# Expert blocks of an attention and mixture-of-experts kernel: x turned by transfers and VectorE in place of TensorE

## The chip, the cores and the metric

One Trainium2 chip, one of its cores. The metric is the time of one execution in microseconds (us), the median of several. PE is TensorE, DVE is VectorE, ACT is ScalarE, POOL is GpSimd, SP is SyncE, which here only issues DMAs.

## What is computed

Attention without softmax, then a dense layer pair, then a routed expert layer:

```python
kv = np.einsum('bhsd,bhse->bhde', k, v)                 # 8 batches, 8 heads, 576 rows, 64 wide
out = np.einsum('bhsd,bhde->bhse', q, kv)
out = out / np.sqrt(np.mean(out * out, -1, keepdims=True) + 1e-06) * g_norm
x = out.transpose(0, 2, 1, 3).reshape(4608, 512)
h = x @ w_in                                            # 512 x 2048
x = (np.maximum(h, 0) + alpha * np.minimum(h, 0)) @ w_out
logits = x @ w_gate                                     # 8 experts
e_idx = np.argmax(logits, axis=1)
for e in range(8):                                      # w1[e] 512 x 1024, w2[e] 1024 x 512
    mask = e_idx == e
    ye = np.maximum(x[mask] @ w1[e], 0) @ w2[e]
    out[mask] = gate_w[mask, None] * eom[mask, e, None] * ye
```

`gate_w` is the softmax weight of the chosen expert and `eom` a sigmoid of a second gate. All is float32. Each product is made of three: an operand is split into a high part, which the matmul's operand type holds, and the rest, and high x high, high x low and low x high are added up.

## The kernel before, in words

**Stages.** Twelve tiles of 384 tokens pass through attention and the dense pair (lines 1334 and 1346 are the latter's matmuls). Each tile writes its rows to `rows` in HBM, 512 values and 16 of metadata a token, and the token's number into the list of its expert (`lists`, line 532). Then come the *expert units*: 128 tokens of one expert each, 41 of them in this execution. Units 0 to 3 are written out one by one, between the last tile's routing and the building of a table (`tab`) of units; units from 4 on run in a hardware loop, two per round (`over_units`, L311), with slots r = 0 and 1.

**A unit.** SP loads 128 token numbers (`uid`, L424). GpSimd gathers these rows into `xrow[:, r]` (L550). PE transposes x in four 128x128 blocks into the PSUM bank psQ (`x_units`, L1429), since the matmul wants the 512 model values on partitions. ACT copies psQ to the high part of `uxT` (L731), DVE subtracts for the low part (L1144) and copies the tokens' gate and number into `umeta` (L1148). `h_unit` (L1448) makes the hidden values in two halves of 512, 12 matmuls each. ACT applies relu (L737), PE transposes h (`h_transpose`, L1458), ACT and DVE split it (`ut`: L742, L1153), and `y_unit` (L1469) adds up y in psAcc0, two halves of 12 matmuls. ACT scales y (L750) and GpSimd scatters the 128 rows to the output (L558).

**Order.** It is written out by hand, the same for all engines. PE's unit u is: h_transpose half 0, h_unit half 1, x_units of unit u+1, y_unit half 0, h_transpose half 1, h_unit half 0 of unit u+1, y_unit half 1. DVE's is ut half 0, ux of u+1 (L1144, L1148), a part of the weights' split (`expert_low`, L966), ut half 1, the other parts. GpSimd's is: wait until x of unit u is transposed and its metadata read, gather for unit u+2, scatter of unit u. Engines meet by semaphores; each engine's instructions start in the order written, so what stands behind a waiting instruction waits too.

**Weights.** An expert's w1 and w2 come in four pieces each of 128x1024 (L406, L409: 512 KB, on SP's queue) into four buffers (`stage2`), and ACT and DVE split them into `W` (L725, L966). w1's piece ch holds the 128 model rows from 128 ch on.

## Time and profile before

| | us |
|---|---|
| three runs, median | 1503.25 |
| lowest and highest | 1499.38, 1505.24 |
| the profiled execution | 1500.92 |
| its span, first to last instruction | 1499.1 |
| PE busy | 1468.6 |
| DVE, ACT, POOL busy | 723.5, 491.3, 127.6 |
| granted clock of TensorE, mean | 0.994 |

The profile is of one execution. Its page gives busy times, a chain of work followed back from the last instruction, and groups of instructions by line; the trace behind it can be asked for a timeline, for one line's instructions and for stretches. Start times count from the first instruction. The rows that count here stand in a section below.

### The profile page before, as it was taken

To read this page: it belongs to the slowest core of one execution; us is meant where nothing else is said; L and a number is where in the kernel's file an instruction comes from. 1 tells how busy PE (TensorE), PEld (TensorE's weight loads), DVE (VectorE), ACT (ScalarE), POOL (GpSimd) and SP (SyncE) were. 2 spreads that over 40 slices of the span, in tenths; PEclk is the share of its full clock that TensorE was granted. 3 is DMA by queue.
4 is the path that set the end of the run, shared out by engine and by line. 5 is a ranking of instruction groups with operands and counts; after the bars stand their busy time and mean duration, and the time that the engine had idled before them with its cause. 6 is when DMAs were issued, how large, how long until landed. Compare 5 with 4: busy or idle time off the path is not lost.

```text
span 1499.1 us, 27268 instructions
## 1 busy us (share of the span) xinstructions
PE 1468.6 (98%) x8553; PEld 1277.5 (85%) x8554; DVE 723.5 (48%) x1796; ACT 491.3 (33%) x994; POOL 127.6 (9%) x143
## 2 busy tenths in 40 slices
PE   7899999999999999999999999999999999999997
PEld 6788989888898989898989898887888888888886
DVE  3585555565656465645555655663122114444411
ACT  3442232323232323223222221433233234444422
POOL 1000000000000000000000000112111111111111
PEclk8999999999999999999999999999999999999999
DMA  8532121102121102213100000524123114444410
GB/s 193 136 95 70 33 75 33 43 2 75 33 75 33 43 2 61 46 36 71 31 13 23 1 22 1 146 88 156 44 91 106 43 37 149 155 142 157 152 41 32
DMA packets 100516, 104.51 MB, mean 70 GB/s; under 512 B 55296, under 2 KB 75920, under 8 KB 100434
## 3 DMA queue, kind: packets, MB, share of 16 engines
q1 hardware_dynamic: 91618, 80.99, 19.6%
q0 software_dynamic: 7872, 21.09, 4.4%
q10 hardware_dynamic: 944, 1.33, 0.4%
q8 instruction: 53, 0.87, 0.3%
q14 instruction: 29, 0.24, 0.1%
HBM read 84.04 MB, written 20.65 MB: 70 GB/s over the span
## 4 chain that ended last, share of the span: by engine, by line
PE 90%; DMA 4%; DVE 2%; ACT 1%; issue 1%; SPq 1%; POOL 0%; ACTq 0%; POOLq 0%; DVEq 0%
PE psAcc L1346 25%; PE psH L1334 24%; PE psAcc L1469 15%; PE psH L1448 14%; PE psO L1458 2%; PE psO L1279 2%; PE psO L1249 1%; PE psQ L1429 1%; PE psQ L1265 1%; DMA AR<-rows,uid 1%; PE psY L1297 1%; DMA lists<-meta,slot 1%; PE psY L1289 1%; PE psY L1306 1%; DMA AR<-in_v_dram 1%
## 5 line engine op out<-in xcount | busy, mean ns | idle before, releaser
L1346 PE MATMUL psAcc<-W,XG 128*128 128x512 f32 x1728 | 438.9, 399 | 0.0
L1334 PE MATMUL psH<-XG,W 128*128 128x384 f32 x2304 | 436.3, 337 | 2.2 <-DVE W L958 1.4
L1334 PEld LDWEIGHTS psH<-XG,W 128*128 128x128 f32 x2304 | 408.4, 188 | 18.0 <-issue 2.7
L1346 PEld LDWEIGHTS psAcc<-W,XG 128*128 128x128 f32 x1728 | 313.7, 188 | 66.1 <-issue 6.0
L683 ACT ACTIVATE XG<-AR 128x128 fp32r<-128x128 f32 (+1 forms) x384 | 132.1, 364 | 639.9 <-DVE AR L988 634.2
L985 DVE TENSOR_SCALAR AR<-psH,acol 128x384 f32<-128x384 f32 x192 | 118.4, 617 | 296.0 <-PE psH L1334 296.0
L1448 PE MATMUL psH<-W,XG 128*128 (+1 forms) x996 | 250.4, 400 | 0.0
L1469 PE MATMUL psAcc<-W,XG 128*128 (+1 forms) x984 | 243.4, 396 | 0.0
L1469 PEld LDWEIGHTS psAcc<-W,XG 128*128 128x128 f32 x984 | 182.9, 189 | 37.3
L1448 PEld LDWEIGHTS psH<-W,XG 128*128 128x128 f32 x996 | 180.8, 188 | 36.8 <-DVE W L966 0.4
L1153 DVE TENSOR_TENSOR XG<-psO,XG 128x512 fp32r<-128x512 f32 x82 | 56.6, 690 | 222.1 <-ACT XG L742 218.8
L992 DVE TENSOR_TENSOR XG<-AR,XG 128x128 fp32r<-128x128 f32 (+1 forms) x384 | 138.0, 359 | 37.4 <-ACT XG L683 0.8
L988 DVE SCALAR_TENSOR_TENSOR AR<-psH,AR 128x128 f32<-128x128 f32 (+1 forms) x384 | 119.2, 352 | 6.6
L532 POOL DMA_INDIRECT lists<-meta,slot x36 | 35.2, 978 | 889.5 <-DVE slot L936 742.6
L737 ACT ACTIVATE AR<-psH 128x512 f32<-128x512 f32 x83 | 49.7, 599 | 142.4 <-PE psH L1448 142.3
L966 DVE TENSOR_TENSOR W<-AR,W 128x1024 f32 (+1 forms) x64 | 75.5, 1219 | 19.8 <-ACT W L725 19.7
L1144 DVE TENSOR_TENSOR XG<-psQ,XG 128x512 fp32r<-128x512 f32 x42 | 29.0, 691 | 96.1 <-issue 53.1
L742 ACT ACTIVATE XG<-psO 128x512 fp32r<-128x512 f32 x82 | 48.8, 595 | 73.3 <-PE psO L1458 59.8
L558 POOL DMA_INDIRECT out_dram<-AR,umeta x41 | 41.3, 1007 | 355.7 <-ACT AR L750 343.7
L725 ACT ACTIVATE W<-AR 128x1024 f32 (+1 forms) x64 | 64.6, 1051 | 9.2 <-issue 7.3
L750 ACT ACTIVATE AR<-psAcc,umeta 128x512 f32<-128x512 f32 x41 | 28.3, 689 | 90.4 <-PE psAcc L1469 90.4
L550 POOL DMA_INDIRECT AR<-rows,uid x43 | 43.8, 1019 | 103.1 <-DMA uid<-lists 65.9
(200 smaller groups left out, 873.3 us busy)
## 6 DMA issues: line engine op xcount, KB each, us to landing
AR<-in_moe_w_dram SPq DMA_DIRECT2D x68, 512.0 KB, 4.9
AR<-in_k_dram SPq DMA_DIRECT2D x16, 576.0 KB, 5.4
rows<-AR SPq DMA_DIRECT2D x36, 256.0 KB, 2.1
AR<-in_q_dram SPq DMA_DIRECT2D x32, 256.0 KB, 3.1
AR<-in_v_dram SPq DMA_DIRECT2D x14, 576.0 KB, 6.8
AR<-in_moe_w_in_dram SPq DMA_DIRECT2D x16, 256.0 KB, 2.9
AR<-in_moe_w_out_dram SPq DMA_DIRECT2D x16, 256.0 KB, 3.5
AR<-in_v_dram ACTq DMA_DIRECT2D x2, 576.0 KB, 9.3
```

The costliest lines, as they stand in the source:

```text
L683: nc.scalar.activation(gT[:, f % 2, 0, n0:n1], g32[:, f % 2, n0:n1], ACT.Copy).then_inc(g_hi, 1)
L725: nc.scalar.activation(piece_of(group, 0, ch), stage2[:, n, :], ACT.Copy).then_inc(expert_hi, 1)
L737: nc.scalar.activation(h_sb[:, half, :], psH[half][:, :], ACT.Relu).then_inc(uh_set, 1)
L966: V.tensor_tensor(piece_of(group, 1, ch), stage2[:, n, :], piece_of(group, 0, ch).bitcast(F32), ALU.subtract).then_inc(expert_split, 1)
L985: V.tensor_scalar(g, h[:, 0:TILE], 0.0, acol[:, f:f + 1], ALU.min, ALU.mult).then_inc(below_set, 1)
L988: V.scalar_tensor_tensor(out=g[:, n0:n1], in0=h[:, n0:n1], scalar=0.0, in1=g[:, n0:n1], op0=ALU.max, op1=ALU.add).then_inc(g_set, 1)
L992: V.tensor_tensor(gT[:, f % 2, 1, n0:n1], g[:, n0:n1], gT[:, f % 2, 0, n0:n1].bitcast(F32), ALU.subtract).then_inc(g_lo, 1)
L1153: V.tensor_tensor(uhT[:, 1, 4 * half:4 * half + 4, :], psO[:, :].rearrange("p (c n) -> p c n", c=4), uhT[:, 0, 4 * half:4 * half + 4, :].b ...
L1334: mm = pe.matmul(psH[f % 2][:, 0:TILE], w_in_v[:, wp, cc, f * P:(f + 1) * P], xT[:, b, xp, cc, :], start=(cc == 0 and (wp, xp) == PARTS[0] ...
L1346: mm = pe.matmul(psAcc[m][:, :], gT[:, f % 2, gp, m * P:(m + 1) * P], w_out_v[:, wp, f, :], start=(f == 0 and (gp, wp) == PARTS[0]), stop= ...
L1448: mm = pe.matmul(psH[half][:, :], uxT[:, xp, cc, :], W[:, bass.ds(par, 1), wp, cc * F2 + half * 512:cc * F2 + half * 512 + 512], start=(cc ...
L1469: mm = pe.matmul(psAcc[0][:, :], uhT[:, hp, cc, :], W[:, bass.ds(par, 1), wp, CH * F2 + cc * DM:CH * F2 + (cc + 1) * DM], start=(cc == 0 a ...
```

## The change

**What it does.** PE no longer transposes x for units 1 and up. GpSimd, after the gather, stores `xrow[:, r]`'s 512 columns to a new HBM tensor `xs`, waits, and reads them back in four DMAs, one for each 32 partitions ("quad"): block (t, quad) of 32 rows by 128 columns goes to partitions of the quad, columns 128 t on. DVE then transposes all 32x32 blocks in one instruction (L1181 of the new kernel) into `ux32`, which lies in `kvbd`'s memory, free at that time. ACT's copy and DVE's subtraction read `ux32` in place of psQ.

The model rows now lie in another order: partition 32 q + j of block c holds row 128 q + 32 c + j. So w1's pieces are read in the same order, in one DMA each as before, from four blocks of 32 rows. Unit 0's x is still transposed by PE, from a copy made by GpSimd in that column order. The transposes of h stay as they were.

```diff
+    xs = nc.dram_tensor("xs", (2, P, DM), F32).ap()
...
+        ux32, ux_first = kvbd[:, 0, :, :], kvbd[:, 1, :, :]
...
                 if ch < 4:
-                    sp.dma_start(st, w1[bass.ds(e, 1), ch * P:(ch + 1) * P, :].rearrange("e p n -> p (e n)")
+                    sp.dma_start(st, w1.rearrange("e (q c j) n -> c (e q) j n", q=4, c=CH)[ch, bass.ds(4 * e, 4), :, :]
                                  ).then_inc(stage2_in[slot2], 16)
...
+            def exchange(u, r, n):
+
+                pool.wait_ge(gathered[r], 16 * n + 16)
+                pool.sem_inc(pool_passed, 1)
+                pool.dma_start(xs[r, :, :], xrow[:, r, 0:DM]).then_inc(ux_saved[r], 16)
+                pool.wait_ge(ux_saved[r], 16 * (n + r))
+                pool.sem_inc(pool_passed, 1)
+                for quad in range(4):
+                    pool.dma_start(xrow[32 * quad:32 * quad + 32, r, 0:DM].rearrange("p (t n) -> p t n", t=4),
+                                   xs[r, :, P * quad:P * quad + P].rearrange("(t i) n -> i t n", t=4)
+                                   ).then_inc(ux_back[r], 16)
...
-                    pool.wait_ge(ux_tr, u + 1)
+                    if by_pe(u):
+                        pool.wait_ge(ux_tr, u + 1)
+                    else:
+                        pool.wait_ge(ux_turned, u + 1)
                     pool.wait_ge(umeta_set, u + 1)
                     gather(r, n + 1)
+                    exchange(u + 2, r, n + 1)
                 scatter(u, r, n)
...
             gather(0, 0)
             gather(1, 0)
+            pool.wait_ge(gathered[0], 16)
+            pool.sem_inc(pool_passed, 1)
+            nc.gpsimd.tensor_copy(ux_first.rearrange("p c (r i) -> p c r i", r=4),
+                                  xrow[:, 0, 0:DM].rearrange("p (r c i) -> p c r i", r=4, c=CH)).then_inc(ux_first_set, 1)
+            exchange(1, 1, 0)
...
+            def ux_turn(u, r, n):
+
+                dve.wait_ge(ux_back[r], 64 * (n + r))
+                dve.wait_ge(ux_lo, u)
+                V.transpose(out=ux32.rearrange("p c (t i) -> p c t i", t=4),
+                            in_=xrow[:, r, 0:DM].rearrange("p (t c i) -> p c t i", t=4, c=CH)).then_inc(ux_turned, 1)
...
+                if ahead:
+                    ux_turn(u + 1, 1 - r, n + r)
                 ut(u, 0)
...
             def unit(u, r, n, ahead=True):
                 h_transpose(u, 0)
                 h_unit(u, 1)
-                if ahead:
-                    x_units(u + 1, 1 - r, n + r)
                 y_unit(u, 0)
```

In the units that are written out, DVE's `ux_turn` stands just ahead of `ux` and behind the first `ut`; in the loop it is the first thing of the unit. `by_pe(u)` is true for unit 0 alone.

GpSimd's queue in one round of the loop: L550 is the gather, L558 the scatter; before:

```order
L565 REGISTER_ALU
L546 ISA
L550 DMA AR<-rows,uid 128x528
L555 REGISTER_ALU
L558 DMA out_dram<-AR,umeta 4608x512
```

and now, where L560 is the gather, L568 the save, L572 the four block reads and L580 the scatter:

```order
L590 REGISTER_ALU
L556 ISA
L560 DMA AR<-rows,uid 128x528
L568 DMA xs<-AR 128x512
L569 ISA
L572 DMA AR<-xs 32x4x128 x4
L577 REGISTER_ALU
L580 DMA out_dram<-AR,umeta 4608x512
```

Five DMAs have come between the gather and the scatter.

DVE's unit in the loop: L1153 is the split of h (ut), L1144 that of x, L1148 the metadata, L966 a weight piece; before:

```order
L1152 ISA
L1153 TENSOR_TENSOR XG<-psO,XG 128x512
L1143 REGISTER_ALU
L1144 TENSOR_TENSOR XG<-psQ,XG 128x512
L1147 ISA
L1148 COPY umeta<-AR 128x2
L1220 ISA
L1220 TENSOR_LOAD tab_mem
L1220 ISA x2
L1206 COMPARE_AND_BRANCH
```

and now, where L1181 is the block transpose, L1196 ut, L1187 the split of x, L1191 the metadata and L1002 a weight piece:

```order
L1179 ISA
L1180 REGISTER_ALU
L1181 STREAM_TRANSPOSE kvbd<-AR 128x512
L1195 ISA
L1196 TENSOR_TENSOR XG<-psO,XG 128x512
L1186 REGISTER_ALU
L1187 TENSOR_TENSOR XG<-kvbd,XG 128x512
L1190 REGISTER_ALU
L1191 COPY umeta<-AR 128x2
L1269 ISA
L1269 TENSOR_LOAD tab_mem
L1269 ISA x2
```

The block transpose has come ahead of the unit's first ut.

PE in the loop, from the last matmuls of h_unit half 1 (L1448) to the first of y_unit (L1469); before:

```order
L1448 MATMUL psH<-W,XG 128x512 x2
L1423 ISA
L1427 REGISTER_ALU
L1429 MATMUL psQ<-ident,AR 128x128 x4
L1433 TENSOR_LOAD tab_mem
L1433 ISA x2
L1433 TENSOR_LOAD tab_mem
L1433 ISA x2
L1463 ISA
L1469 ISA
L1469 MATMUL psAcc<-W,XG 128x512
```

and now, where L1494 is h_unit and L1515 y_unit:

```order
L1494 MATMUL psH<-W,XG 128x512 x2
L1479 TENSOR_LOAD tab_mem
L1479 ISA x2
L1479 TENSOR_LOAD tab_mem
L1479 ISA x2
L1509 ISA
L1512 REGISTER_ALU
L1515 ISA
L1515 MATMUL psAcc<-W,XG 128x512
```

The four transposes of x between the two are gone.

## Rows read from the trace of the kernel before

**Rows 1.** Page, busy time of each engine, and chain that ended last

```profile
PE 1468.6 (98%) x8553; PEld 1277.5 (85%) x8554; DVE 723.5 (48%) x1796; ACT 491.3 (33%) x994; POOL 127.6 (9%) x143
...
PE 90%; DMA 4%; DVE 2%; ACT 1%; issue 1%; SPq 1%; POOL 0%; ACTq 0%; POOLq 0%; DVEq 0%
```

**Rows 2.** Timeline of one unit: start us, us, engine, line, operation, [idle before]

```profile
1057.23 0.69 ACT L750 ACTIVATE AR<-psAcc,umeta 128x512 f32<-128x512 f32 x1 [2.26 <-PE psAcc L1469]
...
1058.60 0.69 DVE L1153 TENSOR_TENSOR XG<-psO,XG 128x512 fp32r<-128x512 f32 x1 [5.69 <-ACT XG L742]
1058.83 1.01 POOL L558 DMA_INDIRECT out_dram<-AR,umeta  x1 [10.04 <-ACT AR L750]
1059.88 0.58 PEld L1429 LDWEIGHTS psQ<-ident,AR 128*128 128x128 f32 x4
...
1060.14 0.99 POOL L550 DMA_INDIRECT AR<-rows,uid  x1 [0.30 <-issue]
...
1060.43 2.60 PEld L1469 LDWEIGHTS psAcc<-W,XG 128*128 128x128 f32 x12
...
1069.57 0.69 ACT L750 ACTIVATE AR<-psAcc,umeta 128x512 f32<-128x512 f32 x1 [2.26 <-PE psAcc L1469]
```

**Rows 3.** Windows, unit 3 to unit 40: length, busy by engine, PE clock, DMA share, GB/s

```profile
1032.41:1489.48 457.07, 456.90 (x2220) 376.40 (x2218) 135.25 (x197) 176.72 (x270) 73.80 (x74) 1.00 0.31 98
```

**Rows 4.** Instructions of line 1429: duration ns min/median/max, first and last start

```profile
L1429 PE MATMUL psQ<-ident,AR x168: 270/272/329, 964.1 to 1480.3; 128*128 128x128 f32 x168
```

**Rows 5.** Page, DVE groups: count, busy us, mean ns, idle before

```profile
L966 DVE TENSOR_TENSOR W<-AR,W 128x1024 f32 (+1 forms) x64 | 75.5, 1219 | 19.8 <-ACT W L725 19.7
L1144 DVE TENSOR_TENSOR XG<-psQ,XG 128x512 fp32r<-128x512 f32 x42 | 29.0, 691 | 96.1 <-issue 53.1
```

**Rows 6.** POOL groups by line, and landing times of line 550

```profile
L532 POOL DMA_INDIRECT lists<-meta,slot x36 | 35.2, 978 | 889.5 <-DVE slot L936 742.6
...
L558 POOL DMA_INDIRECT out_dram<-AR,umeta x41 | 41.3, 1007 | 355.7 <-ACT AR L750 343.7
...
L550 POOL DMA_INDIRECT AR<-rows,uid x43 | 43.8, 1019 | 103.1 <-DMA uid<-lists 65.9
...
L520 POOL CAST W<-AR 128x512 fp32r<-128x512 f32 x1 | 0.6, 609 | 14.5 <-DMA AR<-in_moe_w_out_dram 14.5
...
DMA to landing us min/median/max: 3.2/3.4/7.4
```

**Rows 7.** DMA issues: KB each, median us to landing; issue time of line 409, ns

```profile
AR<-in_moe_w_dram SPq DMA_DIRECT2D x68, 512.0 KB, 4.9
...
rows<-AR SPq DMA_DIRECT2D x36, 256.0 KB, 2.1
...
L409 SPq DMA_DIRECT2D AR<-in_moe_w_dram x32: 372/376/390, 955.8 to 1402.4; - x32
```

**Rows 8.** Timelines of POOL, SP and PE weight loads, 1000 to 1027 us

```profile
1001.19 0.99 POOL L550 DMA_INDIRECT AR<-rows,uid  x1 [6.12 <-issue]
...
1014.02 2.02 POOL L550 DMA_INDIRECT AR<-rows,uid  x1 [10.52 <-DMA uid<-lists]
...
1012.21 3.50 SPq L409 DMA_DIRECT2D AR<-in_moe_w_dram  x4
...
1021.48 0.42 PEld L1429 LDWEIGHTS psQ<-ident,AR 128*128 128x128 f32 x4 [3.65 <-DMA AR<-rows,uid]
1021.87 4.17 PEld L1469 LDWEIGHTS psAcc<-W,XG 128*128 128x128 f32 x12
...
1026.64 2.59 PEld L1448 LDWEIGHTS psH<-W,XG 128*128 128x128 f32 x12
```

**Rows 9.** Page, DMA queue of SP: packets, MB, share of 16 engines

```profile
q1 hardware_dynamic: 91618, 80.99, 19.6%
```

**Rows 10.** Timelines of SP and ACT: w1 pieces issued, and their first use

```profile
1336.95 4.33 SPq L406 DMA_DIRECT2D AR<-in_moe_w_dram  x4
...
1358.43 2.01 ACT L725 ACTIVATE W<-AR 128x1024 f32 x2 [0.55 <-issue]
```

More of the change, by code:

```diff
@@ L248, in attention_dense_moe_routed_moe @@
         ux_tr = sem("ux_tr")
+        ux_saved = [sem("ux_saved0"), sem("ux_saved1")]
+        ux_back = [sem("ux_back0"), sem("ux_back1")]
+        ux_turned = sem("ux_turned")
+        ux_first_set = sem("ux_first_set")
         ux_hi = sem("ux_hi")
@@ L292, in piece_of, with by_pe @@
                           ch * 1024:(ch + 1) * 1024].rearrange("p r q n -> p (r q n)")
+        def by_pe(u):
+            return isinstance(u, int) and u == 0
         def nxt(i, c):
@@ L728, in ux @@
             def ux(u):
-                act.wait_ge(ux_tr, u + 1)
+                if by_pe(u):
+                    act.wait_ge(ux_tr, u + 1)
+                else:
+                    act.wait_ge(ux_turned, u + 1)
                 act.wait_ge(uh_mm, 2 * u + 1)
-                nc.scalar.activation(uxT[:, 0, :, :], psQ[:, :].rearrange("p (c n) -> p c n", c=CH), ACT.Copy
-                                     ).then_inc(ux_hi, 1)
+                act.sem_inc(act_passed, 1)
+                nc.scalar.activation(uxT[:, 0, :, :], psQ[:, :].rearrange("p (c n) -> p c n", c=CH) if by_pe(u) else ux32,
+                                     ACT.Copy).then_inc(ux_hi, 1)
             def uh(u, half):
@@ L951, in _ @@
             dve.sem_inc(ut_lo, 1)
+            dve.sem_inc(ux_turned, 1)
             def dense_low(f):
@@ L1139, in _ @@
             over_tiles(dve, tile)
+            def ux_turn(u, r, n):
[3 more added lines that the diff above has]
+                            in_=xrow[:, r, 0:DM].rearrange("p (t c i) -> p c t i", t=4, c=CH)).then_inc(ux_turned, 1)
             def ux(u, r, n):
                 dve.wait_ge(ux_hi, u + 1)
-                V.tensor_tensor(uxT[:, 1, :, :], psQ[:, :].rearrange("p (c n) -> p c n", c=CH),
+                V.tensor_tensor(uxT[:, 1, :, :], psQ[:, :].rearrange("p (c n) -> p c n", c=CH) if by_pe(u) else ux32,
                                 uxT[:, 0, :, :].bitcast(F32), ALU.subtract).then_inc(ux_lo, 1)
@@ L1169, in _ @@
             expert_low(1, 3)
+            ux_turn(1, 1, 0)
             dve.wait_ge(lg_mm, 3 * t + TG)
@@ L1179, in _ @@
             table_turns()
+            ux_turn(2, 0, 1)
             ux(2, 0, 1)
@@ L1188, in _ @@
             ut(2, 0)
+            ux_turn(3, 1, 1)
             ux(3, 1, 1)
@@ L1197, in _ @@
             ut(3, 0)
+            ux_turn(4, 0, 2)
             ux(4, 0, 2)
@@ L1410, in side @@
                     if not ahead and s == 15:
-                        x_units(0, 0, 0)
+                        x_first()
                 pe.wait_ge(x_lo, 3 * t + 3)
@@ L1419, in tile, with x_first @@
                 output(t, FC - 1)
-            def x_units(u, r, n):
-                pe.wait_ge(gathered[r], 16 * n + 16)
-                if isinstance(u, int) and u == 0:
-                    pe.wait_ge(qT_set, TG * TILES)
-                else:
-                    pe.wait_ge(ux_lo, u)
+            def x_first():
+                pe.wait_ge(ux_first_set, 1)
+                pe.wait_ge(qT_set, TG * TILES)
                 for cc in range(CH):
-                    mm = pe.transpose(psQ[:, cc * P:(cc + 1) * P], xrow[:, r, cc * P:(cc + 1) * P], ident[:, :])
+                    mm = pe.transpose(psQ[:, cc * P:(cc + 1) * P], ux_first[:, cc, :], ident[:, :])
                 mm.then_inc(ux_tr, 1)
@@ L1504, in _ @@
             h_unit(0, 1)
-            x_units(1, 1, 0)
             y_unit(0, 0)
@@ L1514, in _ @@
             h_unit(2, 1)
-            x_units(3, 1, 1)
             y_unit(2, 0)
```

## The prediction, made before the changed kernel was run

> **What bounds the kernel now.** I read the page first. The time is TensorE's: it is busy for 98% of the span, and the chain of work that ended last is 90% PE [rows 1]. Then I took the part the change touches, the expert units. One unit's timeline [rows 2] reads: the second half of unit v is evacuated by ACT at 1057.23 and that of unit v+1 at 1069.57, 12.34 us later. Between them the weight loads on PE follow each other without a gap: the x transposes start at 1059.88 and the next block, y, at 1060.43, so the four transposes take 0.55 us of PE's order. The windows show that this holds for the whole stage: from the evacuation of unit 3 (1032.41) to that of unit 40 (1489.48) are 37 units in 457.07 us, 12.35 us each, with PE busy for 456.90 and a full clock of 1.00 [rows 3]. Nothing is waited for there. In the same stretch POOL is busy for 73.80 us and DVE for 135.25, so there seems to be room. The question is latency and order, not busy time.
>
> **What is removed.** The transposes of line 1429 are 168, 42 sets of four [rows 4]; one set (unit 0) stays. 41 sets at 0.55 to 0.56 us are 23 us of PE. In the loop it is 37 x 0.56 = 20.7 us, and a unit would take 11.79 us if nothing else came late. This is all there is to gain.
>
> **What is added on DVE and ACT.** A 32x32-block transpose of 128x512 per unit. The trace has none; its nearest rows are the 128x512 operations, 0.69 us on DVE [rows 5]. I take 0.65, with 0.5 to 1.3 as the ends. It is one more of some five DVE operations in 12 us, hidden by DVE's idle time. The subtraction and ACT's copy now read SBUF instead of psQ; a 128x1024 operation from SBUF took 1.22 us, so half of it some 0.61 against 0.69 [rows 5]. Nothing on the path.
>
> What matters is **where the transpose stands**: it is the first thing in DVE's unit, ahead of ut(u,0), and it waits for the transfers that bring back x of unit u+1. Queued behind it are ut(u,0), the subtraction, the copy of umeta and ut(u,1). PE waits for ut(u,0) before y_unit(u,0). That ut ended at 1059.29 (1058.60 + 0.69), and y may start at 1059.88 once the transposes are gone [rows 2]: a slack of 0.6 us, while before an x that was late held only the transposes.
>
> **What is added on GpSimd.** Each unit there was one gather and one scatter. Now the queue runs gather, wait for it, save (256 KB), wait for it, four block reads (64 KB each), and only then the scatter. Prices:
> - issue: every DMA on this queue took 0.98 to 1.02 us in its mean, whether its 128 rows carry 4 bytes (lists), 2112 (gather) or 2048 (scatter) [rows 6], and from scatter start to gather start are 1.31 us (1058.83 to 1060.14) [rows 2], so 0.3 between two. A plain copy of 128 rows isn't in the trace. I take 1.0 + 0.29 = 1.29 each; the lower bound is 0.37 us, an issue on SP's queue, and 0.6 with the gap [rows 7].
> - from issue to landing: gather 3.4 us median, 3.2 to 7.4 [rows 6]; a 256 KB store by SP's queue lands in 2.1 [rows 7]. For save and read back I take 3.0, nearer to the row of the same queue; the ends are 2.1 and 3.4.
> - GpSimd's start after a wait: the evacuation ends at 1057.92 and the scatter starts at 1058.83 [rows 2], so 0.91.
>
> The Trainium skill (DMA: Bandwidth & Descriptors, section Anatomy of one DMA — SWDGE (gpsimd) path) gives 2.0 us plus the bytes at 436 GB/s for a DMA on this path. By it the save would take an estimated 2.6 and a block read 2.15, and the forecast below would be some 15 us lower; no row here shows a plain copy on this queue. The table in the same page's section Issuing engine by pattern gives plain loads and stores to Sync and only indirect ones to GpSimd, which speaks against this change.
>
> **Two loops follow, and the slower one sets the unit.**
> (a) *GpSimd's own round*: scatter to gather 1.31, gather 3.4, wake 0.91, save 3.0, wake 0.91, four issues 4 x 1.29 = 5.16. Sum 14.7 us a unit.
> (b) *The ring over two units*: scatter(v) to gather(v+3) 1.31; the exchange to its last landing L = 3.4 + 0.91 + 3.0 + 0.91 + 3 x 1.29 + 3.0 = 15.1; DVE's transpose and ut with their hand-overs 0.1 + 0.65 + 0.69 + 0.1 = 1.54; PE from the start of y (1060.43) to the evacuation (1069.57) 9.14; evacuation to scatter 1.60 (1057.23 to 1058.83) [rows 2]. 1.31 + 15.1 + 1.54 + 9.14 + 1.60 = 28.7 for two units, 14.35 each.
> So a unit takes 14.7 instead of 12.35, 2.35 more; 37 of them are +87 us. The 0.55 us saved on PE is inside this and lost: PE then has some 2.9 us idle a unit. From (b), the change breaks even where L is 11.1 us and gives its whole gain at L of 10.0 or less.
>
> **Before the loop** there is one place more. Unit 4's x was late already: gather at 1014.02, landed after 7.4 us because four weight loads of 512 KB had been issued at 1012.21, PE idle for 3.65 us until 1021.48; h_unit(4,0) then began at 1026.64 [rows 8]. Now gather(3) at 1001.19 is followed by its exchange, 3.4 + 0.91 + 3.0 + 0.91 + 5.16 = 13.4, so gather(4) starts at 1015.9; + 7.4 + (L - 3.4 = 11.7) = 1035.0; transpose, ACT's copy and DVE's subtraction some 2.2, so 1037.2: + 10.6 us. The exchanges of units 1 to 3 delay less than this and lie in the same chain, as does the new GpSimd copy for unit 0 (0.61 us by its casts of the same size [rows 6]).
>
> **Weight loads.** After 1060 there are 12 groups of four loads. A gather in one took 4.0 us more (7.4 against 3.4). An exchange has three such flights, each exposed: between 0 and 12 x 4 = 48 us; since most flights miss the thick of a load, I take 0.5 us each, 6 us.
>
> **Sum**: 1499.1 + 87 + 10.6 + 6 = 1602.7 us of span; the profiled execution took 1500.92, 1.8 us more than its span, so 1604.5, about **1605**. The median of the three runs shown (1503.25) lies 2.3 us above the profiled one, less than I can resolve.
>
> **Rivals.**
> 1. *The exchange is cheap, but not free.* With 0.9 a step and landings of 2.5, L = 3.4 + 0.91 + 2.5 + 0.91 + 2.7 + 2.5 = 12.9, ring 13.25: 37 x 0.9 = 33, and some 7 at unit 4: 1541. With the lowest rows (0.6 and 2.1) L is 11.2, ring 12.4, about + 2 and + 5: 1508, which is no change. For it: a plain copy needs no indices. Against: the issue price did not move with what the DMA carried [rows 6].
> 2. *Faster: the exchange is hidden.* Place: GpSimd's queue behind scatter(v). It decides at L = 10.0: with 0.3 a step and 2.1 a landing L is 3.4 + 0.91 + 2.1 + 0.91 + 0.9 + 2.1 = 10.3, nearly there. Then 1499.1 - 20.7 + 4.8 + 1.8 = 1485. For it: POOL is 9% busy [rows 1]. Against: it takes prices below all rows of this queue.
> 3. *w1 comes late as well.* The four w1 pieces are now read with the model's rows in another order, as four blocks of 32, so that h's rows agree with the new x. The Trainium skill (DMA: Bandwidth & Descriptors, section Why a DMA increments its semaphore by 16 and not by 1) says that a DMA is spread over as many engines, up to 16, as divide the outermost dimension of both sides; the new one is 4. As a mechanism of this kernel: if each piece ran on four of the 16 engines, then, with 80.99 MB in 19.6% of 16 engines' 1499.1 us [rows 9] (17.2 GB/s per engine), four pieces (2.1 MB) would take 30.5 us. They are issued at 1336.95 and first wanted by ACT at 1358.43, the last some 3.5 us later [rows 10]: 25 us, which grows to 30 at 14.7 us a unit. So the slower loop covers it about, with 0 to 5 us for each of 6 loads and up to 8 at the first expert, whose pieces are wanted 22 us after issue: 1605 to 1640, middle 1625. In a loop that stayed at 12.35 it would cost some 5 x 6 + 8 = 38.
> 4. *The clock.* After the 3.65 us of idle time 12 weight loads took 4.17 us, against 2.60 to 2.62 at full clock [rows 2, 8]. If PE's idle stretches do this in each unit, ring (b) grows by 1.5, to 15.1 a unit: + 15, 1620. In round (a) it is covered.
>
> **Chances.** The forecast with rival 4 inside it 0.60 (1575 to 1640); w1 late on top of it 0.10 (1625 and up to 1670); rival 1 dear end 0.15 (1520 to 1560), its cheap end 0.08 (1500 to 1519, of which 0.04 within 0.5%); rival 2 0.07. Half a per cent is about what a measurement of this kernel can tell from no change. So faster 0.07, same 0.04, slower 0.89. The range from 1515 to 1660 leaves out rival 2, most of the cheap end, and the top of rival 3.
>
> **What the profile after would show.** Right: POOL's idle time is no longer before the scatter but before the save and the block reads, waiting for DMA; gather to gather about 14.7 us; DVE's transpose waits for DMA and stands just ahead of ut; PE idle 2 to 3 us before each y block, half 0; unit 4's h block near 1037. Five new DMAs at 1.0 us each would make the busy time of POOL rise by some 210 us (42 exchanges). Wrong: block reads issued every 0.3 to 0.6 us, or landings of 2.1, or GpSimd waiting for ACT before its scatter as now. If ACT waits for w1 pieces, or weight landings rise well over 4.9 us, it is rival 3; a granted clock under 1.00 in the loop is rival 4.

## The result, and the profile after

The changed kernel takes **1714.55 us** (median; 1712.08 to 1717.05) against 1504.24 (1499.38 to 1506.82) of the kernel before on the same chip: 1.1401 times as long, 95% interval 1.1381 to 1.1421, + 210 us. The forecast was 1605, its range 1515 to 1660. The sign was right; the size was not: the time lies outside the range, and above 1670 too, the top of the dearest rival.

The page of the kernel after, with the lines that answer [rows 1, 4, 5, 6, 7, 9]: busy time, the queues, the chain, groups of instructions (count, busy us, mean ns, idle before), and DMA issues. L1181 is the block transpose, L568 the save, L572 the block reads, L560 the gather, L1515 y_unit, L756 ACT's part of the weights' split:

```profile
PE 1496.0 (87%) x8389; PEld 1288.5 (75%) x8390; DVE 749.7 (44%) x1837; ACT 494.6 (29%) x994; POOL 247.4 (14%) x354
...
q1 hardware_dynamic: 91186, 80.99, 16.8%
...
PE 63%; DMA 18%; issue 8%; DVE 4%; ACT 2%; SPq 2%; POOL 1%; DVEq 0%; ACTq 0%; POOLq 0%
PE psAcc L1395 22%; PE psH L1383 21%; DMA uid<-lists 9%; PE psAcc L1515 7%; PE psH L1494 4%; DMA AR<-rows,uid 3%; DMA xs<-AR 2%; DMA AR<-xs 2%; PE psO L1328 2%; PE psO L1298 1%; POOL AR L572 1%; PE psQ L1314 1%; PE psY L1346 1%; PE psO L1504 1%; PE psY L1338 1%
...
L1181 DVE STREAM_TRANSPOSE kvbd<-AR 128x512 f32<-128x512 f32 x41 | 29.2, 711 | 317.0 <-DMA AR<-xs 317.0
...
L572 POOL DMA_DIRECT2D AR<-xs x168 | 93.2, 562 | 137.9 <-DMA xs<-AR 135.5
...
L560 POOL DMA_INDIRECT AR<-rows,uid x43 | 43.5, 1012 | 200.7 <-DMA uid<-lists 167.3
L756 ACT ACTIVATE W<-AR 128x1024 f32 (+1 forms) x64 | 64.5, 1050 | 13.3 <-DMA AR<-in_moe_w_dram 7.2
...
AR<-in_moe_w_dram SPq DMA_DIRECT2D x68, 512.0 KB
xs<-AR POOLq DMA_DIRECT2D x42, 256.0 KB, 2.8
```

PE has fallen from 98% to 87% of a span of 1710.7 us, and DMA holds 18% of the chain in place of 4%. Half of this is a line of which the forecast does not speak: "DMA uid<-lists", the 0.5 KB of token numbers that a gather needs, with 9% of the chain and 167 us of idle time ahead of L560.

The stage of units 4 to 40, from the evacuation of unit 3 to that of unit 40, in the window that answers [rows 3] (length, busy of PE, PEld, DVE, ACT, POOL, clock, DMA share, GB/s):

```profile
1071.12:1701.39 630.27, 476.61 (x2072) 381.95 (x2070) 158.49 (x234) 179.78 (x271) 180.52 (x260) 0.88 0.32 103
```

630.27 / 37 = 17.03 us a unit against 12.35; the stage begins 38.7 us later (1071.12 against 1032.41) and lasts 173.2 longer. The units are not alike: many take 11.8 to 13.5 us, those beside weight loads up to 30.

**A quiet stretch.** Two units with no weight load near them, from the timeline:

```profile
1245.37 0.69 ACT L785 ACTIVATE AR<-psAcc,umeta 128x512 f32<-128x512 f32 x1 [2.26 <-PE psAcc L1515]
...
1246.99 1.05 POOL L580 DMA_INDIRECT out_dram<-AR,umeta  x1 [4.70 <-ACT AR L785]
...
1248.35 1.02 POOL L560 DMA_INDIRECT AR<-rows,uid  x1 [0.30 <-issue]
...
1252.40 0.59 POOL L568 DMA_DIRECT2D xs<-AR  x1 [3.03 <-DMA AR<-rows,uid]
...
1255.91 2.22 POOL L572 DMA_DIRECT2D AR<-xs  x4 [2.93 <-DMA xs<-AR]
...
1259.90 0.71 DVE L1181 STREAM_TRANSPOSE kvbd<-AR 128x512 f32<-128x512 f32 x1 [6.97 <-DMA AR<-xs]
...
1261.57 2.58 PEld L1515 LDWEIGHTS psAcc<-W,XG 128*128 128x128 f32 x12 [1.72 <-issue]
...
1270.74 0.69 ACT L785 ACTIVATE AR<-psAcc,umeta 128x512 f32<-128x512 f32 x1 [2.32 <-PE psAcc L1515]
```

This is the forecast's ring (b): evacuation to scatter 1.62, scatter to gather 1.36, the exchange (gather's issue to the transpose) L = 11.55, transpose to y 1.67, y to the evacuation 9.17; 25.37 us for two units, 12.69 each. The four block reads are issued in 2.22 us, not 5.16. After the idle 1.72 us the twelve weight loads of the y block take 2.58 us, as before [rows 2]: in a quiet unit the stall costs no clock.

**A stretch with a w1 load.** POOL's and SP's queues:

```profile
1193.20 7.62 SPq L416 DMA_DIRECT2D AR<-in_moe_w_dram  x4
1202.52 23.16 SPq L434 DMA_DIRECT2D uid<-lists  x3
...
1202.54 1.05 POOL L580 DMA_INDIRECT out_dram<-AR,umeta  x1 [5.03 <-ACT AR L785]
1221.04 1.02 POOL L560 DMA_INDIRECT AR<-rows,uid  x1 [17.45 <-DMA uid<-lists]
```

The ids are issued at 1202.52, behind the four pieces of w1, and their gather starts at 1221.04: 512 bytes that land in 2.7 us in the median took some 18. The windows show what w1's pieces do meanwhile. First five of after beside the load issued at 1406.52, then the two of before over the load issued at 1336.95 [rows 10]:

```profile
1405.00:1410.00 5.00, 5.00 (x23) 3.93 (x22) 4.90 (x5) 3.06 (x5) 0.59 (x2) 1.00 0.35 97
1410.00:1415.00 5.00, 3.37 (x17) 2.51 (x15) 0.33 (x1) 1.77 (x3) 0.00 (x0) 1.00 0.31 121
1415.00:1420.00 5.00, 0.00 (x0) 0.00 (x0) 0.00 (x0) 0.00 (x0) 3.27 (x5) 0.60 0.41 125
1420.00:1425.00 5.00, 0.00 (x0) 0.00 (x0) 1.29 (x2) 0.55 (x1) 0.00 (x0) 0.50 0.38 139
1425.00:1430.00 5.00, 4.81 (x12) 3.81 (x13) 0.77 (x2) 0.08 (x1) 0.00 (x0) 0.53 0.26 105
```

```profile
1336.00:1341.00 5.00, 5.00 (x24) 4.05 (x23) 4.78 (x5) 2.97 (x4) 0.00 (x0) 1.00 0.76 192
1341.00:1346.00 5.00, 5.00 (x28) 4.17 (x27) 1.13 (x2) 2.26 (x4) 1.01 (x1) 1.00 0.90 326
```

Before, 0.76 to 0.90 of the 16 DMA engines worked, at up to 326 GB/s, and the load was over in some 10 us. Now it is 0.26 to 0.41 of them, the exchange's own transfers included, for over 20 us, and PE stands idle from 1413 to 1425. This is what few engines per transfer would look like; e3 below shows it without the exchange. The Trainium skill (DMA: Bandwidth & Descriptors, section Why a DMA increments its semaphore by 16 and not by 1) has a DMA spread over the largest number of engines, up to 16, that divides the outermost dimension of both sides, here 4 and 128, so 4 of 16; the shares of these windows and of e3's (0.27) agree with it.

### The profile page after: what moved, and what is told of

The parts are those of the page before. It is cut to its first block, busy times and chain, and to the rows that moved or that the text cites. A ratio compares the mean times of both kernels' runs of the same rounds, so it can differ in the third digit from the quotient of the medians.

```text
span 1710.7 us, 27370 instructions
## 1 busy us (share of the span) xinstructions
PE 1496.0 (87%) x8389; PEld 1288.5 (75%) x8390; DVE 749.7 (44%) x1837; ACT 494.6 (29%) x994; POOL 247.4 (14%) x354
## 4 chain that ended last, share of the span: by engine, by line
PE 63%; DMA 18%; issue 8%; DVE 4%; ACT 2%; SPq 2%; POOL 1%; DVEq 0%; ACTq 0%; POOLq 0%
PE psAcc L1395 22%; PE psH L1383 21%; DMA uid<-lists 9%; PE psAcc L1515 7%; PE psH L1494 4%; DMA AR<-rows,uid 3%; DMA xs<-AR 2%; DMA AR<-xs 2%; PE psO L1328 2%; PE psO L1298 1%; POOL AR L572 1%; PE psQ L1314 1%; PE psY L1346 1%; PE psO L1504 1%; PE psY L1338 1%
## 5 line engine op out<-in xcount | busy, mean ns | idle before, releaser
L1515 PE MATMUL psAcc<-W,XG 128*128 (+1 forms) x984 | 269.6, 428 | 154.1 <-DVE XG L1196 154.1
L1395 PEld LDWEIGHTS psAcc<-W,XG 128*128 128x128 f32 x1728 | 316.4, 190 | 70.9 <-issue 6.0
L1515 PEld LDWEIGHTS psAcc<-W,XG 128*128 128x128 f32 x984 | 203.5, 210 | 209.7 <-issue 165.7
L1494 PE MATMUL psH<-W,XG 128*128 (+1 forms) x996 | 255.4, 406 | 13.0 <-issue 13.0
L1494 PEld LDWEIGHTS psH<-W,XG 128*128 128x128 f32 x996 | 185.2, 193 | 51.5 <-issue 14.1
L1181 DVE STREAM_TRANSPOSE kvbd<-AR 128x512 f32<-128x512 f32 x41 | 29.2, 711 | 317.0 <-DMA AR<-xs 317.0
L572 POOL DMA_DIRECT2D AR<-xs x168 | 93.2, 562 | 137.9 <-DMA xs<-AR 135.5
L1196 DVE TENSOR_TENSOR XG<-psO,XG 128x512 fp32r<-128x512 f32 x82 | 55.5, 677 | 123.0 <-ACT XG L777 122.9
L1002 DVE TENSOR_TENSOR W<-AR,W 128x1024 f32 (+1 forms) x64 | 75.6, 1220 | 29.2 <-ACT W L756 29.1
L560 POOL DMA_INDIRECT AR<-rows,uid x43 | 43.5, 1012 | 200.7 <-DMA uid<-lists 167.3
L756 ACT ACTIVATE W<-AR 128x1024 f32 (+1 forms) x64 | 64.5, 1050 | 13.3 <-DMA AR<-in_moe_w_dram 7.2
L766 ACT ACTIVATE XG<-kvbd 128x512 fp32r<-128x512 f32 x41 | 25.7, 626 | 141.2 <-DVE kvbd L1181 141.2
```

The costliest lines, as they stand in the source:

```text
L572: pool.dma_start(xrow[32 * quad:32 * quad + 32, r, 0:DM].rearrange("p (t n) -> p t n", t=4), xs[r, :, P * quad:P * quad + P].rearrange("(t ...
L756: nc.scalar.activation(piece_of(group, 0, ch), stage2[:, n, :], ACT.Copy).then_inc(expert_hi, 1)
L1002: V.tensor_tensor(piece_of(group, 1, ch), stage2[:, n, :], piece_of(group, 0, ch).bitcast(F32), ALU.subtract).then_inc(expert_split, 1)
L1196: V.tensor_tensor(uhT[:, 1, 4 * half:4 * half + 4, :], psO[:, :].rearrange("p (c n) -> p c n", c=4), uhT[:, 0, 4 * half:4 * half + 4, :].b ...
L1395: mm = pe.matmul(psAcc[m][:, :], gT[:, f % 2, gp, m * P:(m + 1) * P], w_out_v[:, wp, f, :], start=(f == 0 and (gp, wp) == PARTS[0]), stop= ...
L1494: mm = pe.matmul(psH[half][:, :], uxT[:, xp, cc, :], W[:, bass.ds(par, 1), wp, cc * F2 + half * 512:cc * F2 + half * 512 + 512], start=(cc ...
```

## The experiments

The evacuation of unit 3 ("unit 3 at") is the start of the stage, and (unit 40 - unit 3) / 37 "a unit". Two profiled executions of code that is the same up to the loop differ in that start by 1 to 3 us (1032.41 before, 1035.34 in e10; 1052.01 in e5, 1049.54 in e9), so of a start some 3 us say nothing. The kernel before was timed beside each group of experiments, with medians of 1499.86 to 1505.09; a ratio is against that neighbour, and where two groups are compared the difference of the ratios is given as well.

### Each half of the change by itself

The w1 load as before, with the exchange kept (e1), and the kernel before with nothing but the new w1 load (e3):

```diff
-                    sp.dma_start(st, w1.rearrange("e (q c j) n -> c (e q) j n", q=4, c=CH)[ch, bass.ds(4 * e, 4), :, :]
+                    sp.dma_start(st, w1[bass.ds(e, 1), ch * P:(ch + 1) * P, :].rearrange("e p n -> p (e n)")
```

> The changed kernel, with w1's pieces loaded as in the kernel before (128 rows in a row, one outer dimension of 128). The rows of w1 then don't match the order of x, so this changes what the expert blocks compute; the work is otherwise the same. Theory A (the new w1 load occupies few DMA engines, and the loads of the 128 token numbers queue behind it on SP's queue): the waits of the gather for the token numbers, 167 us in 12 waits, fall to some 10 us, and a loop unit settles at the ring of 12.6 to 12.8 us that the undisturbed units of the changed kernel show (scatters at 1246.99, 1258.86, 1272.36, 1284.60 and 1297.99), so 1504 + 37 x 0.35 = 1517, plus 5 to 12 at the units before the loop: 1520 to 1530. Theory B (the exchange itself, its two more flights and five more issues, is the price): over 1650.

> The kernel before with nothing but w1's pieces loaded as in the changed kernel, from four blocks of 32 rows. x is not in that order there, so this changes what the expert blocks compute. Theory A: the load of the token numbers behind a w1 load takes some 18 us (in the changed kernel it was issued at 1202.52 and the gather began at 1221.04), against a slack of some 8 us ahead of the x transposes, so each of the six w1 groups in the loop costs 8 to 12 us and the two before it some 10 together: 1504 + 60 to 80 = 1565 to 1585. Theory B: the load is hidden, 1504.

e1: 1603.55 us (1596.55 to 1607.14), ratio 1.0672 [1.0636, 1.0708]; unit 3 at 1049.15, 14.76 us a unit. e3: 1612.94 (1610.05 to 1613.68), ratio 1.0744 [1.0723, 1.0764]; unit 3 at 1055.69, also 14.76 a unit, but as 12.35 in most units and 22 to 25.6 at the w1 loads. So the exchange alone costs + 104, the load alone + 113, and the two together + 210: they add up (0.0672 + 0.0744 against 0.1401 in the ratios). Neither theory of e1 held: 1603.55 lies between 1520 to 1530 and 1650. The expectation that w1 was nearly all of the loss fell, and e3 costs more than its 1565 to 1585.

e3's queues, SP and POOL, show w1's harm without any exchange:

```profile
1162.23 4.96 SPq L406 DMA_DIRECT2D AR<-in_moe_w_dram  x4
...
1187.77 0.99 POOL L550 DMA_INDIRECT AR<-rows,uid  x1 [19.00 <-DMA uid<-lists]
```

And its windows while that load runs:

```profile
1170.00:1175.00 5.00, 5.00 (x25) 4.11 (x24) 0.86 (x2) 1.25 (x3) 0.00 (x0) 1.00 0.27 105
1175.00:1180.00 5.00, 4.08 (x20) 3.08 (x19) 0.69 (x1) 0.60 (x2) 0.00 (x0) 1.00 0.27 105
...
1185.00:1190.00 5.00, 0.00 (x0) 0.00 (x0) 0.00 (x0) 0.00 (x0) 1.93 (x2) 0.81 0.15 32
```

The four pieces, issued from 1162.23 on, move at 105 GB/s with 0.27 of the engines busy, and the traffic falls off only after 1185: some 24 us from issue, in place of some 10. The ids behind them arrive at the end of it, and PE stands idle.

### The same change with w1 read on all engines

If GpSimd's and DVE's reads take every fourth model value in place of a run of 32, partition p of block c holds row 4p + c, and w1's piece is again one dimension of 128 rows. The whole result is computed.

```diff
-                    sp.dma_start(st, w1.rearrange("e (q c j) n -> c (e q) j n", q=4, c=CH)[ch, bass.ds(4 * e, 4), :, :]
+                    sp.dma_start(st, w1.rearrange("e (p c) n -> c e p n", c=CH)[ch, bass.ds(e, 1), :, :].rearrange("e p n -> p (e n)")
...
-                            in_=xrow[:, r, 0:DM].rearrange("p (t c i) -> p c t i", t=4, c=CH)).then_inc(ux_turned, 1)
+                            in_=xrow[:, r, 0:DM].rearrange("p (t i c) -> p c t i", t=4, c=CH)).then_inc(ux_turned, 1)
```

> The changed kernel with a w1 piece made of every fourth row (partition p of piece c holds row 4 p + c): one outer dimension of 128, and DVE's block transpose and GpSimd's first copy read their columns with a step of four elements in place of one, so that x and w1 agree again. Both theories expect of it what they expect of w1's rows as before: A 1520 to 1530, B over 1650. If the strided read makes DVE's transpose longer (0.71 us now), by up to twice, the ring grows by half of that a unit: up to 13 us more in all.

1610.93 us (1608.98 to 1613.26), ratio 1.0741 [1.0721, 1.0761], 14.80 a unit, w1 and w2 landing in 4.7 us (median; 4.9 in [rows 7]). So the order of model rows which the exchange needs can be had without w1's load in blocks: 104 us less than the changed kernel, of the 111 that e1 gains by leaving the order wrong. The other 7 go with DVE's strided read:

```profile
L1181 DVE STREAM_TRANSPOSE kvbd<-AR x41: 1074/1083/1109, 983.7 to 1586.7; 128x512 f32<-128x512 f32 x41
```

### How much of w1's harm is the ids behind it

The changed kernel, but in the loop ACT's queue issues the ids.

```diff
+                if ahead:
+                    act.wait_ge(gathered[r], 16 * n + 16)
...
+                    act.dma_start(uid[:, r:r + 1], lists[bass.ds(at_list, P), :]).then_inc(ids_in[r], 16)
```

> The changed kernel, with the loop's loads of the token numbers (0.5 KB each) issued by ACT on its own queue at the start of its unit, in place of SP. The w1 loads stay as changed. Theory A1 (the token numbers wait in SP's queue behind w1): the gather no longer waits for them (127 us in the loop's ten waits now), and the time falls by 100 to 127 us plus the full clock's share: 1580 to 1610. Theory A2 (a w1 load slows everything that touches its DMA engines, whichever queue): the token numbers still arrive late, and the time stays above 1680.

1673.66 us (1672.29 to 1674.74), ratio 1.1156 [1.1137, 1.1175]. Its waits in the loop (us in total, times, longest):

```profile
DVE kvbd L1182 <- DMA AR<-xs: 259.5, 35, 16.2
POOL xs L564 <- DMA AR<-rows,uid: 134.1, 36, 7.0
POOL AR L568 <- DMA xs<-AR: 131.9, 38, 7.8
```

GpSimd's waits for ids shrink from 116 us (longest 19.4) to 43 (longest 5.2), and 41 us of the 111 come back (37 by the ratios). The time lies between the two theories, and each holds in part. The other 70 remain with another wait: GpSimd waits up to 7.0 us for a gather and 7.8 for a save, and DVE up to 16.2 for the reads. Moving the small load to a free queue moved the place of the wait more than it removed it.

### The exchange's 104 us: flights beside the weight loads, or the loop itself

e1 again, with every weight load of the loop a quarter of its size.

```diff
+                if not isinstance(n, int):
+                    if ch < 4:
+                        sp.dma_start(st[:, 0:F2 // 4], w1[bass.ds(e, 1), ch * P:(ch + 1) * P, 0:F2 // 4].rearrange(
...
```

> The kernel with w1's rows as before and, in the loop, weight pieces of 128 KB in place of 512 KB (the first quarter of the columns of each piece; the rest of the buffer keeps what it held, so this leaves out part of the weights, beside the mismatched order of w1's rows). ACT's and DVE's splits, all waits and all other loads are unchanged. Theory C: the exchange's flights are lengthened by the 2 MB of a weight group, so with a quarter of it the units beside a group, 17 to 20 us now, fall to 12.5 to 14, the mean from 14.76 to about 12.9: 1604 - 37 x 1.85 = 1535. Rival E (the extra time beside a weight group comes from the split's work on ACT and DVE and its order, not from DMA traffic): 1590 to 1604.

1552.1 us (1549.39 to 1552.2), ratio 1.032 [1.0297, 1.0342], 13.27 a unit: 52 us less (53 by the ratios). The split's work and its order are unchanged, and the units beside a group fall from 17 to 20 us to 12.8 to 14.1, but for the first of the loop (19.5) and one of 17.1. So rival E falls; theory C's 1535 was 17 us too low. The control is the kernel before with the same cut:

> This is the kernel before in which the weight loads of the loop bring a quarter of each piece (128 KB in place of 512 KB); three quarters of each weight piece are missing, so the result is not the reference's. It is the control for e6 and e9. Theory C: the kernel before has only one flight a unit (the gather), asked for more than a unit ahead, so it hides the weight traffic already and gains nothing: 1497 to 1505, units at 12.35. Rival H (the weight loads cost any version some time, also without the exchange, so that the 52 us which e6 gained are not the exchange's alone): 1470 to 1490.

1501.64 (1498.54 to 1503.84), ratio 1.0003 [0.9986, 1.0019]. The kernel before gains nothing, so the weights' bytes cost these 52 us only where the exchange is present. Most of that goes through the exchange's own flights; GpSimd's waits for the ids in the loop fall too, from 20.1 us in e1 to 10.4 in e6, and their part was not measured apart. In e1 one such place reads (PE's weight loads, POOL, SP, DVE):

```profile
1279.04 5.21 SPq L419 DMA_DIRECT2D AR<-in_moe_w_dram  x4
...
1282.94 2.23 POOL L572 DMA_DIRECT2D AR<-xs  x4 [3.54 <-DMA xs<-AR]
...
1290.97 0.71 DVE L1181 STREAM_TRANSPOSE kvbd<-AR 128x512 f32<-128x512 f32 x1 [7.25 <-DMA AR<-xs]
...
1292.61 4.76 PEld L1515 LDWEIGHTS psAcc<-W,XG 128*128 128x128 f32 x12 [5.16 <-issue]
```

The reads need 8.0 us from first issue to transpose (4.0 in the quiet stretch), PE waits 5.2 us, and its next twelve weight loads take 4.76 in place of 2.60 [rows 2], as those after the stall in [rows 8] did (4.17). The granted clock there is in the windows of e1:

```profile
1287.00:1292.00 5.00, 0.87 (x4) 0.38 (x2) 1.03 (x2) 0.72 (x2) 0.68 (x2) 0.89 0.58 187
1292.00:1297.00 5.00, 4.39 (x10) 3.46 (x11) 2.25 (x4) 2.52 (x3) 1.44 (x2) 0.50 0.19 54
```

PE's idle time in the first window is followed by a clock at its lower level, 1.2 GHz, in the second.

### The transpose behind the first ut

e2 with DVE's transpose one step later in the loop, so that a late x no longer holds `ut(u, 0)`, which PE's y block needs.

```diff
-                if ahead:
-                    ux_turn(u + 1, 1 - r, n + r)
                 ut(u, 0)
...
+                ux_turn(u + 1, 1 - r, n + r)
                 ux(u + 1, 1 - r, n + r)
```

> The kernel with w1 in every fourth row, and DVE's block transpose moved in the loop from ahead of ut half 0 to behind it, just ahead of the split of x. Theory C (the transfers that bring x back are late, and what they cost is set by where the waiting instruction stands): x is then wanted some 3.3 us later (h_unit half 0 in place of y_unit half 0), ring (b) loses its ut and its first y block and falls under PE's own 11.8 us, so undisturbed units take 11.8 to 12.0 us (12.75 in the kernel with w1's rows as before) and units beside a weight load, 17 to 20 us there, some 4 us less: mean near 13.3, 1530 to 1560. Rival D (GpSimd's own round, 1.36 + 4.05 + 3.5 + 2.5 = 11.4 us plus its waits, is what holds the units): no more than 10 us are gained, 1600.

1573.3 us (1570.1 to 1574.53), ratio 1.0465 [1.0439, 1.049], 37.6 less than e2 (41 by the ratios). Quiet units now take 11.87 us: nearly the full gain, which the forecast put at 11.79. Beside weight loads they still take 15 to 19, so the mean is 13.76 and the time lies above the expected 1530 to 1560. The same kernel with quarter weight loads asks what is left without them:

> This is the kernel of e5 (exchange, w1 taken as every fourth row, DVE's transpose behind the first ut) in which the weight loads of the loop bring a quarter of each piece (128 KB in place of 512 KB); three quarters of each weight piece are missing, so the result is not the reference's. Theory C (what e5 still loses in the loop is the exchange's flights lengthened by the bytes of the weight loads): the loop starts as in e5 (unit 3's last evacuation at 1052) and its 37 units take 11.87 us where nothing crosses them, and about 12.4 in the mean, since e6 kept some 0.6 us a unit above its own undisturbed 12.7: 37 x 12.4 = 459, 1511 + 11 = 1500 to 1525, no slower than 2% over the kernel before. Rival G (what is lost beside the weight loads is order and not bytes: ids issued behind four weight loads in SP's queue, ACT and DVE splitting weights): the units beside loads stay at 15 to 19 us and the time at 1555 to 1575.

1524.87 us (1522.59 to 1530.45), ratio 1.0172 [1.0129, 1.0215], 12.49 a unit, as theory C had it. The stage is within 5 us of before (37 x 0.13); the rest of the + 24 is the start, unit 3 at 1049.54, 17 us late. So even with three quarters of the weight traffic gone the exchange gains nothing here.

### The exchange issued by another queue

e5 with the save and the reads issued by ACT in the loop, so that GpSimd never waits for them.

```diff
+            def save(r, n):
+                act.wait_ge(gathered[r], 16 * n + 32)
...
+            def read_back(r, n):
+                act.wait_ge(act_saved[r], 16 * (n - 1 + r))
```

> The kernel with the late block transpose, and in the loop the save and the four block reads issued by ACT on its own queue: the save behind ut half 1 (by when the gather should have landed), the reads behind the relu of half 0, so that GpSimd's round is gather and scatter again. L falls by the issues (0.37 in place of 0.56 us), by GpSimd's two waits of some 0.6 us and by the shorter landing (2.1 for a 256 KB store on SP's queue). Theory C: undisturbed units take 11.8 us, those beside a weight load 12 to 14, mean 12.3 or less, 1500 to 1520; the exchange before the loop still costs its 15 us. Rival F (ACT, held by waits for DMA, delays the evacuations of psH and psAcc): no gain over the late transpose alone, or slower than it.

1603.45 us (1602.37 to 1605.65), ratio 1.0668 [1.0644, 1.0691], 30 worse than e5, as rival F had it. ACT's own work now queues behind the transfers:

```profile
1298.72 1.02 POOL L582 DMA_INDIRECT out_dram<-AR,umeta  x1 [11.89 <-ACT AR L788]
1303.56 0.60 ACT L780 ACTIVATE XG<-psO 128x512 fp32r<-128x512 f32 x1 [5.76 <-DMA AR<-xs]
```

L780 is ACT's ut, of which PE's y block waits. ACT has work that PE needs, so here a wait for a transfer costs more on its queue than on GpSimd's.

### The 17 us before the loop

In e1 DVE's, SP's and POOL's rows at units 2 to 4 show a dependence that the forecast missed (the first row is the gather of unit 3):

```profile
1005.93 0.99 POOL L560 DMA_INDIRECT AR<-rows,uid  x1 [6.31 <-issue]
...
1016.87 0.71 DVE L1181 STREAM_TRANSPOSE kvbd<-AR 128x512 f32<-128x512 f32 x1 [10.03 <-DMA AR<-xs]
...
1020.50 0.15 DVE L1173 CAST tcol<-tei 128x1 f32<-128x1 int32 x1
...
1023.72 0.33 SPq L434 DMA_DIRECT2D uid<-lists  x1
...
1026.60 1.01 POOL L560 DMA_INDIRECT AR<-rows,uid  x1 [10.13 <-DMA uid<-lists]
```

DVE waits 10 us for x of unit 3. Behind this wait stand the last steps of the table of units, and the ids of unit 4 are read at an offset from that table: unit 4's gather comes at 1026.60 in place of 1014.02 [rows 8]. Two versions of e5 take the table out from behind the wait, first its computing steps, then also the copy of the finished table (with ACT's and DVE's `ut(2, 1)`); DVE's part of the second, against e5:

```diff
+            table_experts()
             ut(2, 0)
-            ux_turn(3, 1, 1)
-            ux(3, 1, 1)
-            table_experts()
             ut(2, 1)
             dve.wait_ge(tab_mm, 1)
             V.tensor_copy(tab[:, :, :], psY[0:1, 0:FIELDS * COLS].rearrange("p (f u) -> p f u", f=FIELDS)
                           ).then_inc(tab_set, 1)
+            ux_turn(3, 1, 1)
+            ux(3, 1, 1)
```

> This is the kernel of e5 with one call moved: DVE's last steps of the table of units (table_experts, which end in tcol_set) stand ahead of ut(2,0) and the transpose of x of unit 3, not behind them. The whole result is computed. Where the start of the loop is late was not in the forecast's terms: in e1 DVE waits 10.0 us for x of unit 3 (transpose at 1016.87), the table's last steps behind it end at 1020.65 in place of 1008.23 before, the ids of unit 4 are issued at 1023.72 in place of 1011.11, and its gather at 1026.60 in place of 1014.02. Theory T (the table held by the wait accounts for the late gather of unit 4): the ids go out near 1012, the gather follows GpSimd's scatter of unit 2 and the transpose of unit 3 at about 1018, the last evacuation of unit 3 moves from 1052 to about 1044 and the whole to 1562 to 1568. Rival S (GpSimd's own queue holds that gather all the same, as the forecast's sum of 1015.9 plus flights had it, and the saving is lost to the weight loads that come earlier too): unit 3 at 1050 or later and 1570 to 1576.

> This is the kernel of e5 in which, for unit 2, nothing of the table of units stands behind the transpose of x of unit 3: DVE does the table's last steps, ut(2,0), ut(2,1) and the copy of the finished table (tab_set), and only then waits for x; ACT's ut(2,1) stands ahead of its copy of x for the same reason. e11 moved the table's steps alone, its copy still stood behind the transpose, and the gather of unit 4 came only 2 us earlier against unit 3's transpose. The whole result is computed. Theory T: the ids of unit 4 are issued within 2 us of 1013, its gather follows the transpose of unit 3 (some 1017) by about a microsecond instead of 8 to 10, the last evacuation of unit 3 moves to 1042 to 1046 and the whole to 1562 to 1568. Rival S (GpSimd's queue holds it all the same): unit 3 at 1049 or later and 1568 to 1574.

e11 (`table_experts()` alone): 1569.21 (1564.42 to 1571.97), ratio 1.0465 [1.0435, 1.0495], the same ratio as e5; unit 3 at 1049.32. The copy still stood behind the transpose, so the ids went out at 1022.17, and the run doesn't tell the theories apart. e12: 1568.23 (1566.28 to 1569.94), ratio 1.0423 [1.0403, 1.0444], the fastest version that computes the whole result; unit 3 at 1042.97. POOL's and SP's rows of e12:

```profile
1017.07 0.33 SPq L434 DMA_DIRECT2D uid<-lists  x1
...
1020.00 1.01 POOL L560 DMA_INDIRECT AR<-rows,uid  x1 [0.38 <-issue]
```

The gather follows the scatter with no wait for ids, and unit 3 ends 9 us earlier than in e5, as theory T said. Of these some 5 us reach the end (6 by the ratios, whose intervals just overlap, so it is hardly resolved), and 1568.23 lies on the border between the two theories: it is the rows that decide for T. The stage itself takes 13.84 a unit against 13.76 in e5 and 13.62 in e11; why was not measured. The other 10.6 us of the late start (1042.97 against 1032.41) remain. A part is there one gather earlier, behind the exchanges of units 1 and 2: that of unit 3 starts at 1008.80 in e12 and at 1005.93 in e1, in place of 1001.19 [rows 8] (1003.73 in e10). What each of the early exchanges costs was not taken apart.

## Why the forecast was right or wrong

Two steps failed. The one that put the time out of the range is w1's load on four engines: the sum gave it nothing, since "the slower loop covers it about", and it measured 104 to 113 us. The other is the term for the exchange's flights beside weight loads, 6 us in the sum and 52 or more in the runs. It was masked by a loop term that was too dear.

**What bounds the kernel, and what is removed: right.** PE was the bound and the transposes were worth 0.5 us a unit: quiet units of e5 take 11.87 where 11.79 was given.

**Prices of the exchange: too dear.** A block read's issue was put at 1.29 us with its gap, from the indirect DMAs; it is 0.56 (548 to 603 ns). The lower bound, 0.6, was the right end. A save was put at 3.0 us to landing; the median is 2.8. The Trainium skill's fit (DMA: Bandwidth & Descriptors, section Anatomy of one DMA — SWDGE (gpsimd) path) gave an estimated 2.6, a little below that median and within 2.3 to 7.6. DVE's transpose was put at 0.65; it is 0.711. L is 11.55, not 15.1, and most of the difference is in the block reads: 3.99 us from first issue to the transpose, where the forecast had 6.87 to the last landing. POOL's busy time rose by 120 us, not 210.

**The two loops: the mechanism right, the size wrong.** With the measured L, the forecast's other terms of ring (b) (1.31, 1.54, 9.14, 1.60) give 12.57 a unit, and the quiet stretch has 12.69. So the ring adds 0.34 a unit, between the two ends of rival 1 (13.25 and 12.4). Round (a), the slower loop of the forecast, is 11.87 us in the quiet stretch (scatter 1246.99 to scatter 1258.86), the last 0.73 of it spent waiting ahead of the scatter, and does not set the pace. The term of + 87 us should have been some 13.

**The exchange's flights beside weight loads: a step that failed.** The term was 6 us, 0.5 a flight, because "most flights miss the thick of a load". The runs show 52 us and more (e1 against e6, with the control e10). Where flights one after another take 11.5 us of a unit of 12.7, there is no gap that a load of some 10 us could fall in, and each lengthened flight reaches PE at once. Then the clock falls as well, as rival 4 had it, though only after the longer stalls: after 1.72 us of idle time in the quiet stretch twelve weight loads took 2.58 us, after 5.16 us in e1 they took 4.76. The bound of 48 us stood in the forecast; it was not an outer end but about the value.

**Before the loop: + 10.6 forecast, + 17 measured** (e1). The gather's delay was put down to GpSimd's own queue, the gather at 1015.9. It came at 1026.60, since the table waits behind DVE's new wait. The forecast said what is queued behind the transpose in the loop, and did not ask the same of the written-out units. It also gave the exchanges of units 1 to 3 nothing of their own, and the gather of unit 3 was 4.7 us later in e1 than before (2.2 later than in e10).

**Rival 3, w1 on four engines: the larger failure. It happened, was given 0.10, and was priced by the wrong waiter.** The forecast asked when ACT would want w1's pieces, and found 0 to 5 us each. In that it was right: ACT waited for weights only 7.2 us in all (L756 above). What was hurt were the other transfers in flight: the ids behind it in SP's queue (41 us by e4) and the exchange's other transfers (70). Alone it costs 113 us at a loop of 12.35 (e3), where the forecast had 38; the ids behind w1 are what GpSimd waits for there, 19.00 us in the place shown. The rule stood in the forecast, and a duration of the load of 30.5 us; e3's windows show some 24, at 105 GB/s, or some 26 GB/s an engine if four carry it, where the forecast had 17.2. The step missing was: who else uses these engines and this queue during these 20 to 25 us?

**Why the sum looked good for e1.** e1 took 1603.55, nearly the forecast's 1605 without rival 3. That is two errors that cancel: 87 for the loop in place of some 13, and 6 for the weight loads in place of 52 and more. It is no support for the sum. The + 104 of e1 are: 17 before the loop; 52 which the three quarters of the weight bytes account for; and 35 (13.27 - 12.35 = 0.92 a unit, 34) of which the ring's 0.34 a unit is 13 and the rest lies mostly in the first unit of the loop (19.5 in e6) and in the units that meet the quarter loads, and was not taken apart.

**Open.** What part of the 52 us is the exchange's longer flights, what part the later ids, and what part the lower clock after the stalls was not measured apart. e1's mean granted clock was 0.966 and e6's 0.982; both fall and rise with the stalls.

## What to carry to other kernels

Before replacing 0.5 us of a busy engine by a chain of transfers, close the ring: add the latencies from the release of the buffer to its next use, and compare with the ring's period. Where the transfers fill the period, as here 11.5 us of 12.7, other traffic that lengthens them reaches the critical path, and "most of them miss" is no estimate. When a DMA's access pattern changes, price it by what else flies and queues while it runs, not only by who wants its data, and look for an order of rows that keeps a long outermost dimension (here every fourth row in place of four blocks: 104 us). When an instruction that can wait is put into a hand-written order, list what stands behind it in every place where it was put, not only in the loop.

## What the runs showed of the hardware that was not expected

- A plain 64 KB DMA on GpSimd's queue is issued in 0.56 us and a 256 KB one in 0.59, against 1.01 for the indirect gather. The price of 1.0 us was that of the indirect form here.
- DVE's block transpose of 128x512 takes 0.711 us where it reads runs of 32 values, and 1.083 where it reads every fourth.
- A 0.5 KB load took 18 us where it stood in one queue behind four loads of 512 KB which kept some 0.27 of the DMA engines busy (e3). Issued from ACT's queue its gather waited at most 5.2 us.
